# A dynamic convolution with a gated feed-forward: fewer warm-up transposes, gains on another queue, two reordered feature blocks, a later wait and a shifted tile

## The reference

```
w = exp(weight_gen - max(weight_gen, -1));  w = w / (sum(w, -1) + 1e-09)
out[b, s, h] = sum_k w[b, s, h, k] * x_pad[b, s + k, h]        # x_pad: six zero rows ahead, groups of 24 columns per head
x = out.reshape(16384, 192)
xn = x / sqrt(mean(x * x, -1) + 1e-06) * rms_g
g = xn @ w_gate;  val = xn @ w_val
return (g / (1 + exp(-g)) * val) @ w_out
```

## Time and profile before

| | us |
|---|---|
| median of 3 runs (lowest, highest) | 1303.09 (1302.23, 1303.92) |
| the profiled execution | 1302.11 |
| its span, first to last instruction | 1300.2 |
| PEld, VectorE, ScalarE, GpSimd busy | 1191.3, 1003.4, 662.8, 44.7 |
| idle before up-projection matmuls (w_hi), before output matmuls (h_hi) | 3.6, 5.2 |
| HBM read, written | 38.06 MB, 12.58 MB |

### The profile page before, as it was taken

The page is one execution under the profiler, slowest core; times in us unless marked ns, Lnnn a source line. Parts: engine busy times, 40 slices in busy tenths (PEclk is TensorE's granted clock), DMA queues, the critical chain, the costliest instruction groups (busy, mean ns, idle before and its releaser), DMA issues.

```text
span 1300.2 us, 32479 instructions
## 1 busy us (share of the span) xinstructions
PE 1282.3 (99%) x13544; PEld 1191.3 (92%) x13544; DVE 1003.4 (77%) x1516; ACT 662.8 (51%) x1426; POOL 44.7 (3%) x75
## 2 busy tenths in 40 slices
PE   8999999999999999999999999999999999999998
PEld 6888888899999888888889999999999999999998
DVE  6998888777787787787877777777777877877643
ACT  4554555565445555445564455554455554455543
POOL 1000000000000000000000000000000000000000
PEclk8999999999999999999999999999999999999999
DMA  9011321211211212212212112111112121121010
GB/s 298 28 40 29 96 65 43 68 58 53 63 47 53 68 44 68 56 38 68 68 44 68 51 43 68 53 59 56 46 60 68 45 67 56 38 68 38 14 38 14
DMA packets 19734, 76.29 MB, mean 59 GB/s; under 512 B 3212, under 2 KB 4876, under 8 KB 19464
## 3 DMA queue, kind: packets, MB, share of 16 engines
q1 hardware_dynamic: 18764, 72.78, 18.8%
q10 hardware_dynamic: 828, 1.47, 0.5%
HBM read 38.06 MB, written 12.58 MB: 39 GB/s over the span
## 4 chain that ended last, share of the span: by engine, by line
PE 92%; DVE 2%; ACT 2%; issue 2%; DMA 1%; ACTq 0%; POOL 0%
PE up_ps L795 59%; PE out_ps L835 22%; PE out_ps L839 10%; DMA raw<-in_moe_w_val 1%; DVE h L682 1%; PE up_ps L744 1%; DVE h_lo L702 1%; ACT silu L468 0%; ACT L448 0%; DVE prod L223 0%; ACT L468 0%; DVE y L225 0%; PE up_ps L749 0%; DMA taps<-in_weight_gen 0%; DVE last L634 0%
## 5 line engine op out<-in xcount | busy, mean ns | idle before, releaser
L795 PE MATMUL up_ps<-xT,w_hi 64*128 64x512 f32 x4608 | 789.0, 394 | 3.6 <-DVE h L682 2.8
L795 PEld LDWEIGHTS up_ps<-xT,w_hi 64*128 64x128 f32 x4608 | 482.2, 184 | 57.5 <-issue 6.1
L795 PE MATMUL up_ps<-xT,w_lo 64*128 64x512 f32 x2304 | 480.7, 392 | 0.0
L835 PE MATMUL out_ps<-wo,h_hi 64*128 64x384 f32 x3072 | 459.2, 355 | 5.2 <-ACT silu L468 1.5
L682 DVE TENSOR_TENSOR h<-up_ps,silu 128x512 f32<-128x512 f32 x384 | 264.7, 689 | 211.1 <-ACT silu L468 211.0
L839 PE MATMUL out_ps<-wo,h_lo 64*128 64x192 f32 x3072 | 418.1, 247 | 0.0
L483 ACT ACTIVATE h_hi<-h 128x512 fp32r<-128x512 f32 x384 | 242.4, 631 | 332.3 <-DVE h L682 332.3
L468 ACT ACTIVATE silu<-up_ps 128x512 f32<-128x512 f32 x384 | 228.6, 595 | 265.1 <-PE up_ps L795 252.3
L835 PEld LDWEIGHTS out_ps<-wo,h_hi 64*128 64x128 f32 x3072 | 321.2, 184 | 11.1 <-DVE last L634 2.3
L839 PEld LDWEIGHTS out_ps<-wo,h_lo 64*128 64x128 f32 x3072 | 325.7, 187 | 3.3
L702 DVE TENSOR_TENSOR h_lo<-h,h_hi 128x512 fp32r<-128x512 f32 x384 | 263.2, 686 | 35.3 <-ACT h_hi L483 35.0
(11 more groups left out here) (75 smaller groups left out, 301.1 us busy)
## 6 DMA issues: line engine op xcount, KB each, us to landing
x_buf<-in_x SPq DMA_DIRECT2D x30, 960.0 KB, 4.7
xT<-xT SPq DMA_DIRECT2D x90, 256.0 KB, 3.8
result<-last SPq DMA_DIRECT2D x32, 384.0 KB, 2.3
taps<-in_weight_gen SPq DMA_DIRECT2D x1, 3136.0 KB, 20.9
raw<-in_moe_w_gate SPq DMA_DIRECT2D x3, 384.0 KB, 8.9
raw<-in_moe_w_val ACTq DMA_DIRECT2D x3, 384.0 KB, 10.6
last<-in_moe_w_out SPq DMA_DIRECT2D x1, 1152.0 KB, 18.3
x_first<-in_x SPq DMA_DIRECT2D x2, 384.0 KB, 7.4
```

The lines of the kernel that those rows point to most:

```text
L795: mm = nc.tensor.matmul(ps[:, banks, :], w[rows, s, cols], xT[rows, t, s, part, :], start=(at == 0), stop=ends)
L835: nc.tensor.matmul(out_ps[:, j, 0:2 * D], h_hi[rows, g % HB, cols], wo[rows, g, :, :].rearrange("p a d -> p (a d)"), start=(g == 0 and k < ...
```

## The change

- `WARM_TURNS` goes from 50 to 34.
- The gains are loaded from SP's queue, by three DMAs behind the first part of x and ahead of the first w_gate (before: five DMAs on ScalarE's queue, behind the first w_val). On ScalarE's queue the first w_val goes ahead of the exponential of the first taps.
- In token blocks 0 and 1, `hidden` takes a part: high steps of f = 0, high steps of f = 1, low steps of f = 0, low steps of f = 1. In block 0 the high steps of f = 1 wait for the first x_lo, whose source they overwrite.
- TensorE's wait for silu, h and xn before a turn stands behind part k = 0 of the projection instead of ahead of it. Block 1: VectorE's scaling of xn goes ahead of the mix steps of f = 8. Block 2: ScalarE's scaling is done in f = 7 in two halves, ahead of and behind h_hi, instead of behind h_hi of f = 7 and of f = 8.
- A tile `spare` of 16 bytes a partition stands ahead of `xn`, and tiles start at multiples of 32: `xn`, `xT`, `silu`, `h`, `h_hi` and `h_lo` move up by 32 bytes. In the built program `xT` starts at byte 175584 of a partition instead of 175552.

```diff
+        spare = sb("spare", [P, J])
...
-        WARM_TURNS, KEEP_TURNS = 50, 30
+        WARM_TURNS, KEEP_TURNS = 34, 30
...
             load_first(0)
+            with nc.allow_non_contiguous_dma(reason="192 gains, one to a partition"):
+                chunks = g_d.rearrange("(s c) a -> c (s a)", c=DB)
+                sp.dma_start(gains[0:DB, :], chunks).then_inc(gains_loaded, 16)
+                sp.dma_start(gains[DB:P, 0:SLOTS:2], chunks[:, 1:SLOTS]).then_inc(gains_loaded, 16)
+                sp.dma_start(gains[DB:P, 1:2], chunks[:, 0:1]).then_inc(gains_loaded, 16)
             load_w(0)
...
-            first_exps(0)
...
             load_val(0)
-            act.dma_start(gains[:, 0:1], g_d[0:P, :]).then_inc(gains_loaded, 16)
-            for s in (1, 2):
-                for m in range(2):
-                    c = CHUNKS[m][s]
-                    act.dma_start(gains[m * DB:(m + 1) * DB, s:s + 1], g_d[c * DB:(c + 1) * DB, :]).then_inc(gains_loaded, 16)
+            first_exps(0)
             load_val(1)
             load_val(2)
...
-                squares_at, scales_at = ((0, 1), (2, 3)) if T > 3 else ((), {2: (7, 8), 3: (4, 5)}.get(T, ()))
-                squares_early, scales_early = {0: 10, 1: 7, 2: 6, 3: 3}.get(T), {0: 11, 1: 8}.get(T)
+                squares_at, scales_at = ((0, 1), (2, 3)) if T > 3 else ((), {3: (4, 5)}.get(T, ()))
+                squares_early, scales_early = {0: 10, 1: 7, 2: 6, 3: 3}.get(T), {0: 11, 1: 8, 2: 7}.get(T)
...
+                    if T == 2 and f == scales_early:
+                        scale(T + 1, 1 - t, range(J // 2, J))
...
+                    if T == 1 and f == 8:
+                        scale_rest(2, 0)
                     if mixes:
                         for c, n in steps_of(T, f):
                             mix_waits(c, n)
                             mix(c, c % 2, n)
                     if first and f == xf:
                         scale_rest(1, 1)
-                    if T == 1 and f == 8:
-                        scale_rest(2, 0)
...
-            def hidden(T, t, f):
+            def hidden(T, t, f, part=None):
...
                 steps = [(s, n) for s in range(SLOTS) for n in range(3)]
-                if T < 2 and f == 0:
-                    steps.sort(key=lambda at: at[1] == 2)
+                first, last = steps[0], steps[-1]
+                if part is not None:
+                    steps = [(s, n) for s, n in steps if (n == 2) == (part == 1)]
...
+                if first and f == 1:
+                    pe.wait_ge(x_lo_done, 1)
...
                     project_two(T, f, k)
                     if k == 0 and turned is not None:
+                        pe.wait_ge(silu_done, FB * T + turn_after(T))
+                        pe.wait_ge(h_done, FB * T + turn_after(T))
+                        pe.wait_ge(xn_done, 2 * J * (T + 2))
                         turn_x(T + 1, 1 - turned, pair(turned, f + 4))
...
                     hidden_waits(T, f, first)
+                    if T < 2 and f == 0:
+                        hidden(T, t, 0, 0)
+                        hidden_waits(T, 1, first)
+                        hidden(T, t, 1, 0)
+                        hidden(T, t, 0, 1)
+                        hidden(T, t, 1, 1)
+                        continue
                     hidden(T, t, f)
...
-                    if f + 1 == xf and not (first or last):
-                        pe.wait_ge(silu_done, FB * T + xf)
-                        pe.wait_ge(h_done, FB * T + xf)
-                        pe.wait_ge(xn_done, 2 * J * (T + 2))
```

More of the change, by code:

```diff
@@ L377, in w_high @@
                     if s == 0:
-                        act.wait_ge(gains_loaded, 80)
+                        act.wait_ge(gains_loaded, 48)
                     act.wait_ge(w_loaded[s], 32)
@@ L774, in first_wait @@
                         pe.wait_ge(end_lo_moved, T + 1)
-            def hidden(T, t, f):
+            def hidden(T, t, f, part=None):
                 banks = pair(t, step_of(f, turn_after(T)))
                 cols = slice(f * P, (f + 1) * P)
-                parts = ((w_hi, 0), (w_lo, 0), (w_hi, 1))
                 steps = [(s, n) for s in range(SLOTS) for n in range(3)]
-                if T < 2 and f == 0:
-                    steps.sort(key=lambda at: at[1] == 2)
-                for at, (s, n) in enumerate(steps):
-                    w, part = parts[n]
+                first, last = steps[0], steps[-1]
+                if part is not None:
+                    steps = [(s, n) for s, n in steps if (n == 2) == (part == 1)]
+                for s, n in steps:
+                    w, half = ((w_hi, 0), (w_lo, 0), (w_hi, 1))[n]
                     if T < 2 and f == 0:
@@ L791, in hidden @@
                         pe.wait_ge(x_copied, 48 * (T - 1))
-                    ends = at == len(steps) - 1
                     for m, (ps, done) in enumerate(((gate_ps, gate_done), (val_ps, val_done))):
                         rows = slice(m * DB, (m + 1) * DB)
-                        mm = nc.tensor.matmul(ps[:, banks, :], w[rows, s, cols], xT[rows, t, s, part, :],
-                                              start=(at == 0), stop=ends)
-                        if ends:
+                        mm = nc.tensor.matmul(ps[:, banks, :], w[rows, s, cols], xT[rows, t, s, half, :],
+                                              start=((s, n) == first), stop=((s, n) == last))
+                        if (s, n) == last:
                             mm.then_inc(done, 1)
```

## The result

The changed kernel takes 1292.25 us (1290.67 to 1293.05, four runs), the kernel before 1302.67 on the same chip: ratio 0.9919, 95% interval 0.9906 to 0.9931, some 10 us less. The page of the changed kernel gives a span of 1291.4 us, with TensorE busy for 98% of it.

The account below looks back on a forecast made before the run. TensorE, busy 99% of the span, was taken as the bound, leaving its idle time and wrong-clock time to win. Terms -3.25 + 1.40 - 1.60 - 1.10 = -4.55 us gave 1298.5 us, range 1295.8 to 1302.9.

Parts of the forecast that it names:

- xT 32 bytes higher: Tile places in the up projection: moving xT by 32 bytes was put at nothing in the sum.
- F: Rival, up-projection pairs: a faster read of xT at its new place, 3.5 us per ns a pair; chance 0.04.
- E: Rival, up-projection pairs: tiles 32 bytes off a multiple of 64 read slower, 1308.9 us at 3 ns a pair; chance 0.08.
- The opening: Start through token block 0: first up matmul 2.20 us earlier, then -0.14 and -0.91 at full clock, sum -3.25 us.
- The landing term: Opening: the last weight lands at 18.9 us, the middle between 16.8 at best and 21.1 as before.
- Case D: Rival, opening: weights land at 21.1 as before because SP's w_gate loses what w_val gains; 1302.8 us, chance 0.16.
- B: Rival, opening: TensorE's clock falls to half all the same, total -2.5, 1300.6 us; chance 0.22.
- The reordering in block 0: Feature blocks 0 and 1, token block 0: -0.14 - 0.91 us at full clock, a cost of 1.0 at half clock.
- The reordering in block 1: Feature blocks 0 and 1, token block 1: gate 0 and VectorE's chain shift later, +1.40 us.
- The turns: TensorE's wait before the turn goes behind the first output part: -1.6 us in token block 1, -1.1 in block 2.
- Warm-up: Opening: sixteen fewer warm-up transposes let the sums start earlier; saves nothing by itself, the sums are not on the chain.
- A: The forecast itself: weights landing between 17.5 and 20.3 give 1297.1 to 1299.9 us; chance 0.40.

Follow-up runs that it names:

- experiments 1: The kernel before with the 16-byte spare tile alone, nothing else changed: 1292.92 us, ratio 0.9929.
- experiment 2: The changed kernel without the spare tile: 1300.89 us, ratio 0.9981.
- 4: The kernel before with xn and xT 32 bytes higher, and silu, h, h_hi and h_lo 64 bytes higher: 1293.01 us, ratio 0.9925.
- experiment 10: The changed kernel with the steps of feature blocks 0 and 1 in the old order: 1289.56 us, ratio to the kernel before 0.9901.
- experiment 12: The changed kernel with 50 warm-up transposes: 1292.41 us, ratio to the kernel before 0.992.
- number 6: The kernel before with xn, xT and all behind 64 bytes higher: 1304.33 us, ratio 1.0017.
- numbers 8: The kernel before with a spare tile between w_hi and w_lo, so w_lo, wo, xT and all behind are 32 bytes higher: 1297.84 us, ratio 0.9962.
- 13: The kernel before with the spare tile and the turn's parts alone: 1289.59 us, ratio 0.9902.

## Why the prediction was wrong

- **xT 32 bytes higher: the step that failed.** I put this term of the sum at nothing; a faster read had a chance of 0.04 (F) and a slower one 0.08 (E), and the range left out both. It measured 18 pairs in 4.16 instead of 4.21 us, about 3 ns a pair, 9 to 10 us (experiments 1, 2 and 4). The price per ns, 3.5 us, was right; its size and sign were not. The argument against it, that wo's matmuls show no other overhead, compared another pair of operands and told nothing of this one. The row needed was not in any trace: an up pair at another place. Taken at 3 ns to both sides, E's own example, the range would have begun near 1288.
- **The opening, -3.25 forecast, +1.6 measured** (the second stretch at 39.42 by the timeline of the changed kernel, 37.83 before). The landing term failed, a second wrong step: instead of 18.9 the third w_hi started at 21.54. Case D, 21.1, was it, and the clock was at half as in B; D's sum had that in it. What I had counted as bytes at 225 GB/s ran at 201, and w_gate, pushed behind the gains, landed 12.5 us after its issue in the median, 8.9 before. The last w_val of the kernel before did need 11.90 us, but my reading "its row held little" was wrong: it held two more w_val and the five gains loads, 384 pieces of four bytes that took about 10 us from issue to landing. The change put such pieces ahead of w_gate (the three loads landed 5.9, 7.0 and 8.6 us after issue), and a sum of bytes leaves them out. The trace fits this; no run has the gains moved without w_val. The Trainium skill, DMA: Bandwidth & Descriptors, "Queues, rings and completion order", has an engine take packets in turn from the queue rows that have work. The order that I worked out from it, w_val early and w_gate last, is that of the trace (7.8 and 12.5 us from issue to landing); the best-case time for the last one is not.
- **The reordering in block 0.** Case D worked it out as +1.0 at the half clock; measured +1.25 (1.59 less the 0.34 of the start).
- **The reordering in block 1, +1.40.** Measured +1.35 between the traces (1.56 us behind the kernel before at the start of the block, 2.91 at f = 4), and 2.7 for both blocks in experiment 10 against 1.0 + 1.4. The three waits stand where they were put; that before the output part is 0.90 instead of near 1.1.
- **The turns, -1.6 and -1.1.** Measured between the traces: block 1 from 2.80 us behind the kernel before at f = 8 to 1.17 at f = 10 (-1.6), block 2 from 1.10 to -0.12 (-1.2, of which 0.1 is the pace). Right.
- **Warm-up, at nothing, and the first sum at 7.65**: right (experiment 12, and 7.76). That all six sums would move by 1.57 us failed with the late x.
- Without the tile the forecast of case D was 1302.8, and experiment 2 gave 1300.9, a little better than that and less good than A. With -9.6 for the tile the sum would have been 1288.9, 3.4 us below the measured time: that is the opening. The term at "nothing" is larger than all the others measured together.

## What to carry over

In a loop that one engine fills to 99%, look first at its commonest instruction: 3 ns a pair were worth more here than all the waits that were worked on. Try a few placements of the streamed operand against the stationary one, one spare tile each, and read the pace from the length of equal stretches in the chain. When an edit moves addresses, it is an edit of every later instruction; give it a test of its own. And a load that was made earlier on one queue was paid for on the other here, with the DMA engines at 0.87 to 0.91: sum what must be in, count small pieces too and not only bytes, and ask which transfer is last then. Before a clock is explained by one execution, look whether another kernel's trace shows the same without the edit.

## What the runs showed of the hardware

- The start-to-start distance of fp32r matmul pairs (64 rows, 512 columns) depends on where the streamed tile lies against the weight tiles: 4.16, 4.18, 4.21 or 4.22 us for 18 pairs, with only spare tiles added. 32 bytes made 0.7% of the kernel; moving weights and xT together made none.
- Where the clock falls in the opening differs between executions: the first up pair takes 0.79 us in most traces, 0.50 in that of number 6 behind 3.50 us of idle, and 0.50 with the gap filled by transposes. In all of them the lower level came, filled gap or not (0.50 to 0.70 from 24.7 to 29.9 us).
- The landing of the same loads differs between executions: the first up matmul of kernels with the old opening lay mostly between 24.3 and 25.3 us, and in three profiled executions (numbers 8, 13 and 4) at 26.31, 26.86 and 28.23.
